# Second expert layer: weight loads issued by SyncE, and another order of the weight splits

## What is computed

```
for e in range(E):            # E = 8, N = 3072, D = 320, F = 1024
    mask = expert_idx == e    # expert_idx = argmax(x @ w_gate)
    xe = x[mask]
    h = np.maximum(xe @ w1[e], 0.0)      # w1[e]: 320 x 1024
    ye = h @ w2[e]                       # w2[e]: 1024 x 320
    out[mask] = gate_w[mask, None] * ye
```

## Time and profile before

| | |
|---|---|
| runs | 869.16, 870.5, 877.2 |
| median | 870.5 |
| the profiled execution | 880.63 (span 878.9) |
| mean granted TensorE clock, share of full speed | 0.900 |
| TensorE matmul busy | 729.0 (83%) |
| DVE, POOL, ACT busy | 529.1 (60%), 413.2 (47%), 290.1 (33%) |
| second layer in the trace | 613.8 to 878.9 |

### The profile page before, as it was taken

One profiled execution on the slowest core, in us unless ns is written; L12 is line 12 of the kernel. 1 busy time (PEld: TensorE's weight loads), 2 busy tenths in 40 slices (PEclk: granted clock), 3 DMA queues, 4 the chain that ended last, 5 costly groups with the idle time before them and its releaser, 6 DMA issues. The chain is left out here.

```text
span 878.9 us, 17001 instructions
## 1 busy us (share of the span) xinstructions
PE 729.0 (83%) x5044; PEld 672.5 (77%) x5044; DVE 529.1 (60%) x1622; ACT 290.1 (33%) x756; POOL 413.2 (47%) x557
## 2 busy tenths in 40 slices
PE   0999999994328795986959799983899998999897
PEld 0899999993217684866847698982899997999896
DVE  6479999985775556555556545445546364464462
ACT  4222222220014241422314246451524254245241
POOL 6568878871043452352426375874224043242341
PEclk9999999996558897897779799996899998999999
DMA  8857666625431411223221424535462424623610
GB/s 272 190 148 191 193 186 187 179 79 171 115 130 29 145 48 45 91 87 95 87 73 50 132 66 140 180 105 161 158 206 73 145 70 116 201 81 124 186 33 17
DMA packets 99641, 109.59 MB, mean 125 GB/s; under 512 B 39053, under 2 KB 83726, under 8 KB 99568
## 3 DMA queue, kind: packets, MB, share of 16 engines
q1 hardware_dynamic: 85792, 74.83, 29.8%
q10 hardware_dynamic: 9696, 21.24, 7.5%
q0 software_dynamic: 4080, 12.61, 4.5%
HBM read 89.45 MB, written 20.02 MB: 125 GB/s over the span
## 5 line engine op out<-in xcount | busy, mean ns | idle before, releaser
L535 POOL TENSOR_TENSOR parts_w2l<-all_w,parts_w2h 128x320 fp32r<-128x320 f32 x128 | 113.5, 903 | 131.2 <-ACT parts_w2h L522 128.2
L595 DVE SCALAR_TENSOR_TENSOR l_hl<-bank,l_hh 128x384 fp32r<-128x384 f32 (+1 forms) x168 | 83.1, 494 | 137.6 <-ACT l_hh L591 134.9
L591 ACT ACTIVATE l_hh<-bank 128x384 fp32r<-128x384 f32 (+1 forms) x168 | 74.0, 440 | 167.5 <-PE bank L576 163.0
L572 PE MATMUL bank<-l_xh,parts_w1h 128*128 128x384 f32 x256 | 94.8, 370 | 23.1 <-DVE l_xh L565 12.6
L573 PE MATMUL bank<-l_xl,parts_w1h 128*128 128x384 f32 x256 | 90.0, 352 | 0.0
L574 PE MATMUL bank<-l_xh,parts_w1l 128*128 128x384 f32 x256 | 89.8, 351 | 0.0
L529 POOL TENSOR_TENSOR parts_w1l<-all_w,parts_w1h 128x384 fp32r<-128x384 f32 x72 | 70.3, 1005 | 38.8 <-ACT parts_w1h L515 38.8
L1343 PE MATMUL bank<-parts_w2h,l_hh 128*128 128x320 f32 x192 | 74.4, 387 | 7.1 <-issue 7.1
L582 PE MATMUL bank<-parts_w2h,l_hh 128*128 128x320 f32 x232 | 74.5, 321 | 0.0
L572 PEld LDWEIGHTS bank<-l_xh,parts_w1h 128*128 128x128 f32 x256 | 50.9, 199 | 29.1 <-issue 15.2
L584 PE MATMUL bank<-parts_w2h,l_hl 128*128 128x320 f32 x232 | 71.6, 309 | 0.0
(11 more groups left out here) (253 smaller groups left out, 1900.5 us busy)
## 6 DMA issues: line engine op xcount, KB each, us to landing
all_w<-in_moe_w SPq DMA_DIRECT2D x10, 1280.0 KB, 6.3
all_w<-in_moe_w SPq DMA_DIRECT2D x10, 1024.0 KB
all_w<-in_moe_w ACTq DMA_DIRECT2D x6, 1280.0 KB, 12.5
att_kT<-in_kT SPq DMA_DIRECT2D x24, 256.0 KB, 2.8
att_qD<-in_qT SPq DMA_DIRECT2D x48, 128.0 KB, 3.1
att_qT<-in_qT SPq DMA_DIRECT2D x24, 256.0 KB, 3.1
all_w<-in_moe_w ACTq DMA_DIRECT2D x6, 1024.0 KB
all_w<-in_moe_w SPq DMA_DIRECT2D x20, 256.0 KB
```

The costliest lines, as they stand in the source:

```text
L535: ops.tensor_tensor(sh.w2l[:, r, p, :], sh.w2[:, p, :], sh.w2h[:, r, p, :].bitcast(FP), ALU.subtract).then_inc(sh.w2_low, 1)
L572: T.matmul(dst, sh.w1h[:, r, k, f], xh[:, k, :], start=k == 0, stop=False)
L591: return nc.scalar.activation(hh, src, ACT.Relu)
L595: return nc.vector.scalar_tensor_tensor(hl, src, 0.0, hh.bitcast(FP), ALU.max, ALU.subtract)
```

## The change

SP issues the weight loads of expert e+2 in the first body of expert e: w1 when the low pieces of w1 are all made, then w2 when those of w2 are. ACT issues none. ACT makes the eight pieces of w1 beside the up products, one step later than before, and the eight pieces of w2 between the row tiles in the down products. DVE makes its low pieces of w1 one with every up product and the last two around row tile 0. POOL's low pieces of w2 stand in three groups (4, 2, 2), with one scatter of `y` after each.

```diff
@@ second_layer, sync: body
                     for i in range(1, NE):
                         pad_end(sp, sh, i, padded)
+                if first and e + 2 < NE:
+                    sp.wait_ge(sh.w1_low, FT * (NE + e + 2))
+                    load_w1(sp, sh, a["moe2_w1"][e + 2])
+                    sp.wait_ge(sh.w2_low, FT * (NE + e + 2))
+                    load_w2(sp, sh, a["moe2_w2"][e + 2])
@@ gpsimd: body
-                    if e + 1 < NE:
-                        for p in range(FT):
-                            split_low_w2(nc, pool, nc.gpsimd, sh, NE + e + 1, (e + 1) % 2, p)
-                    for j in range(CT):
+                    for j, pieces in enumerate((range(0, 4), range(4, 6), range(6, FT))):
+                        if e + 1 < NE:
+                            for p in pieces:
+                                split_low_w2(nc, pool, nc.gpsimd, sh, NE + e + 1, (e + 1) % 2, p)
                         pool.wait_ge(y_done, CT * e + j + 1)
@@ scalar: body
-                    if split:
-                        high_w1(e + 1, f)
-                        if f % 2:
-                            high_w2(e + 1, f // 2)
+                    if split and f:
+                        high_w1(e + 1, f - 1)
                 if split:
-                    row_tile(e + 1, 0)
-                    high_w2(e + 1, 4)
-                    row_tile(e + 1, 1)
-                    high_w2(e + 1, 5)
-                    high_w2(e + 1, 6)
-                    row_tile(e + 1, 2)
-                    high_w2(e + 1, 7)
+                    high_w1(e + 1, FT - 1)
+                    for j, pieces in enumerate((range(0, 3), range(3, 6), range(6, FT))):
+                        row_tile(e + 1, j)
+                        for p in pieces:
+                            high_w2(e + 1, p)
                 act.wait_ge(rT_psum, g + 2)
                 rows_high(nc, xh_r, p_T[1], tile(0)).then_inc(rh_done, 1)
-                if split and e + 2 < NE:
-                    act.wait_ge(sh.w1_low, FT * (NE + e + 2))
-                    act.wait_ge(sh.w2_low, FT * (NE + e + 2))
-                    load_w1(act, sh, a["moe2_w1"][e + 2])
-                    load_w2(act, sh, a["moe2_w2"][e + 2])
@@ vector: body
-                    if split and f % 2:
-                        low_w1(e + 1, f // 2)
+                    if split and f > 1:
+                        low_w1(e + 1, f - 2)
                 if split:
+                    low_w1(e + 1, FT - 2)
                     row_tile(e + 1, 0)
-                    low_w1(e + 1, 4)
+                    low_w1(e + 1, FT - 1)
                     row_tile(e + 1, 1)
-                    low_w1(e + 1, 5)
...
                     row_tile(e + 1, 2)
                     tags(e + 1)
-                    low_w1(e + 1, 6)
                 row_tile_r(g)
-                if split:
-                    low_w1(e + 1, 7)
```

## The result

The changed kernel is slower: 883.16 against 871.29, medians of four runs each, ratio 1.0145 with a 95% interval of 1.011 to 1.018. The forecast was 866.0, in a range of 859.5 to 873.0. The sign was wrong. Medians here are over all runs of a kernel, while ratios compare only runs outside a slower state of the chip, so a ratio can differ by up to 0.3% from the quotient of two medians.

The account below looks back on a forecast made before the run. TensorE bound the kernel, stalled 6.58 + 4.12 = 10.7 us by late weight loads in experts 3 and 6. -10.7 + 6.0 = -4.7 against the profiled 880.63 gave 875.9, as a median 865.9; range 859.5 to 873.

Parts of the forecast that it names:

- Earlier loads: First bodies of experts 3 and 6: both weight-load stalls go, -10.7; w2 free 1.4 after TensorE starts the extra tile (T0).
- Splits: Up and down products: ACT's, DVE's and POOL's reordered weight pieces cost nothing, covered by TensorE; uncovered some 0.4 us a piece.
- The new wait: First extra tiles of experts 0, 1, 3 and 4: row load lands behind w2, TensorE waits 1.5 us each, +6.0.
- The upper bound of 2.7 on the wait: Each extra tile's row wait at most 2.7, with w2 landing in 7.2 and both additions doubled.
- rival 2: Waits in the extra tiles lower TensorE's clock, 3.0 more per wait: +7.3, 877.7; chance 0.09.
- order in a queue: SP's queue: transfers move one after the other, so the extra tile's row load waits behind w2; the sum hangs on this.
- rival 1: Extra tiles' small row loads are not held up, all sharing the DMA engines: -10.7, 859.9; chance 0.14.
- Rivals 3: Rows of expert e+2 come too late in experts 3 and 6, 1.5 us each: -1.7, 868.8; chance 0.10.
- 4: Something else, PSUM or the w1 load, holds experts 3 and 6 half as long as before: +0.6, 871.1; chance 0.05.
- the 2 us of cover: Experts without an extra tile: rows of e+2 land at T0 + 9.7, wanted at T0 + 11.7, so cost nothing.

Follow-up runs that it names:

- Experiments 1: Changed kernel, but SP issues the w2 load of expert e+2 at the head of its next first body, behind the extra tiles' row loads: 861.76, ratio 0.986.
- experiment 6: Changed kernel, but POOL makes all eight low pieces of w2 before its first scatter, as in the kernel before: 860.34, ratio 0.987.
- 9: Changed kernel, SP still waiting at w2_low before the extra tile's row load, but w2 itself loaded only at the next first body's head: 862.06, ratio 0.988.
- experiment 7: Changed kernel, but DVE takes the next expert's tags and ids behind the store of the second tile of y: 876.83, ratio 1.005.
- experiment 3: Changed kernel with only half of w2 loaded (640 KB), output not the reference's: 867.79, ratio 0.993.
- Experiment 8: Changed kernel, but ACT issues the w2 load while SP keeps its wait for w2_low, then issues the row load: 882.09, ratio 1.011.

## Why the prediction was wrong

**Earlier loads: right.** The forecast was -10.7 and the two periods gave -11.35. Experiments 1, 6 and 9 confirm it as a total, with layers 11.1 to 11.7 shorter than before.

**Splits: "cost nothing", half wrong.** No wait of TensorE is released by a split, as said (a pause of 0.65 ahead of expert 6's first product has no releaser in the profile and stays open). But the sum treated DVE's and POOL's instructions as independent. POOL's pieces now run beside DVE's cast and held it for 2.0, and the store of the second tile waited behind it. Hence w2 was free at T0 + 2.2 and not at T0 + 1.4 (experiment 7 gives 1.4 without the cast). That is worth 2.3 over the four waits.

**The new wait: right place, wrong size.** Place, count and releaser were as forecast: the first extra tile of experts 0, 1, 3 and 4, released by the row load. The term was +6.0 and measured +21.6:

| | us |
|---|---|
| forecast, 4 x 1.5 | 6.0 |
| w2 free later (experiment 7 against the changed kernel) | 2.3 |
| rows land later than sized, with w2 free on time (waits of 10.37 in experiment 7, less 6.0) | 4.4 |
| clock behind the waits | 9.0 |
| sum (21.6 without the rounding) | 21.7 |

*The landing.* I had added 1.0 to the 6.1 of a lone w2 load. In the changed kernel w2 took 8.1, 7.8, 6.6 and 6.9 to land in the four places, and the rows were there another 0.8 to 1.0 behind it. So the addition held, and what was sized too small is w2's own landing: a time taken from a stretch with an empty queue was used where other transfers move too. In experiment 7 the rows were there 7.7 to 9.4 behind the w2 issue. Which of the other transfers slows w2 is not shown. The 193 KB of rows and a scatter go out beside it in all four places. The 579 KB of further rows follow within 4 us in three of them, but not for expert 1, where w2 took 7.8 all the same:

```profile
all_w<-in_moe_w SPq DMA_DIRECT2D x1, 1280.0 KB, 7.8
parts_raw<-rows SPq DMA_DIRECT2D x1, 160.0 KB
parts_raw<-rows SPq DMA_DIRECT2D x1, 33.0 KB
out<-l_y,l_ids POOLq DMA_INDIRECT x1
```

These are all the transfers issued from 679.4 to 688.5. The upper bound of 2.7 on the wait was also added up wrongly. Its own terms give 1.4 + 7.2 + 1.1 + 0.9 = 10.6, less 7.1, which is 3.5. The waits of 3.97 and 3.53 are beyond even that.

*The clock.* This was rival 2, at 0.09, with 3.0 per wait against the 2.2 measured. I put it aside because a pause of 1.80 in the first layer had left the clock at 1.00. One such pause bounds nothing: in experiment 3 pauses of 1.98 and 1.55 were followed by 0.50, and 0.78 and 0.61 were not. The measured +10.2 is beyond even the +7.3 of that rival, since the waits were twice their size as well. The forecast put the clock behind the waits at nothing, and at 9.0 it is the largest part of the miss.

**Why the forecast's argument was wrong even where its number pointed right.** I had the rows wait in SP's queue behind w2, and took the landings of w1 and w2, 3.3 apart, as evidence for order in a queue. They are just as well explained by two transfers sharing the engines, started 1.7 apart. Experiment 8 settles the point on which the sum hung: with two queues the waits are shorter by 0.1 at most. And rival 1 read the sharing of the engines as "no wait", at 0.14; the sharing is true and the wait is there.

**Rivals 3 and 4 didn't come.** In experts 3 and 6 no first transpose waited; the 2 us of cover held.

**Base.** A change in one layer is read from that layer: the profiled execution of before had spent 7.7 more ahead of it than that of the changed kernel, which made the two spans look alike.

## What to carry to other kernels

When a load is handed to an engine with an in-order queue, list what stands behind its wait, and price that at the stretch where it now lands, with everything else that moves then, not at a lone transfer's time. Let the wait for a buffer stand where nothing with a near deadline is behind it, or free the buffer before the deadline: here either of two small reorderings turned +1.4% into -1.4%. A TensorE wait in a dense stretch should be priced with the clock behind it, here some 1.5 to 3 us for each wait of 1.5 to 4 us for rows.

## What the runs showed that I had not expected

- **Small DVE copies held by POOL.** A cast of 128x3 that took 0.16 to 0.48 before took 1.97 to 2.03 in all seven bodies where POOL's pieces ran beside it, and the 128x2 copy took 1.47 to 1.55 instead of 0.16, while DVE's operations from PSUM (0.42, 0.29 and 0.55) kept their times. The Trainium skill (SBUF — State Buffer, SBUF: two separate sides) describes a pair of SBUF ports that only one of VectorE and GpSimd holds at a time, for a whole instruction, while the other is blocked. Two cases fit one instruction (0.76 for the cast in experiment 6, 0.77 at most for the copy in experiment 7, a piece being about 0.87); the 2.0 spans two pieces and the end of a scatter. Why it was not let in between the pieces there is open.
- **Queues and engines.** Transfers from ACT and SP begun 0.7 to 1.4 apart were as late as in one queue (7.1 to 8.4 for w2 and waits of 2.6 to 3.9).
- **The clock.** Behind waits of 1.55 to 4 in this stretch it fell to 0.50, between 1.1 us before TensorE's restart and 1.0 us behind it, and came back 3.4 to 6.8 us after it fell, in the changed kernel and experiment 3; behind waits of 0.61 and 0.78 it didn't fall.
- **Open.** The rows were later for experts 0 and 1 (waits of 3.97 and 3.53) than for experts 3 and 4 (2.54 and 2.60), and so in every variant with these waits. In the changed kernel it is w2 itself that lands later there (8.1 and 7.8 against 6.6 and 6.9). No run tells why.
